# A convolution and two dense layers on one core: two accumulator readings awaited apart, and both layers' PSUM banks used in turn in the tail

## What is computed

```python
# attention-like part: a causal convolution of 7 taps, softmax weights per head (8 heads of 24 features)
x = attn(x, softmax(weight))                  # (2, 4096, 192) -> 8192 rows of 192
# layer 1
h = x @ w_in1                                 # 192 -> 2048
g = h * sigmoid(1.702 * h)
x = g @ w_out1                                # 2048 -> 192
# layer 2
h = x @ w_in2
P = a0 + a1*h + a2*h^2 + a3*h^3
Q = 1 + |b0|*|h| + |b1|*h^2
out = (P / (Q + 1e-6)) @ w_out2
```

## Time and profile before

| | |
|---|---|
| median of 3 runs | 1399.64 us (1399.02 to 1403.59) |
| the profiled execution's own time | 1398.76 us |
| its span in the trace | 1396.6 us, 2.2 us less than its time |
| PE busy | 1328.7 us, 95% of the span |
| DVE busy | 1107.6 us, 79% |
| ACT busy | 972.0 us, 70% |
| POOL busy | 326.5 us, 23% |

### The profile page before, as it was taken

How to read it: one execution, slowest core, us unless ns; L and a number is a source line. 1 busy time by engine, 2 the same in 40 slices (tenths; PEclk the granted TensorE clock), 3 DMA queues, 4 the chain that set the end, 5 groups by cost and what they waited for, 6 DMA issues and landing times. The chain is left out here.

```text
span 1396.6 us, 14941 instructions
## 1 busy us (share of the span) xinstructions
PE 1328.7 (95%) x4896; PEld 706.6 (51%) x4896; DVE 1107.6 (79%) x1205; ACT 972.0 (70%) x1113; POOL 326.5 (23%) x150
## 2 busy tenths in 40 slices
PE   2999999999999999999999999999999999999886
PEld 1455555554555555555554555555455555555332
DVE  5229788887888888888888888888888888877885
ACT  4337777677777777677777767777677777766774
POOL 4202222222222222222222222222222222222222
PEclk9999999999999999999999999999999999999998
DMA  8100000000000000000000000000000000000000
GB/s 209 36 12 0 12 1 23 1 23 1 12 11 0 23 0 20 3 11 11 0 23 0 12 10 3 20 0 23 0 12 12 0 12 1 12 0 12 0 12 11
DMA packets 32884, 20.37 MB, mean 15 GB/s; under 512 B 10322, under 2 KB 30802, under 8 KB 32850
## 3 DMA queue, kind: packets, MB, share of 16 engines
q1 hardware_dynamic: 32372, 19.93, 5.2%
q10 hardware_dynamic: 477, 0.01, 0.0%
HBM read 13.64 MB, written 6.29 MB: 14 GB/s over the span
## 5 line engine op out<-in xcount | busy, mean ns | idle before, releaser
L675 POOL TENSOR_TENSOR work<-work 128x1024 f32<-128x1024 f32 x128 | 303.7, 2373 | 1013.2 <-ACT work L432 1010.1
L271 PE MATMUL acc_a<-g,down 128*128 128x512 f32 x1024 | 477.4, 607 | 0.0
L271 PEld LDWEIGHTS acc_a<-g,down 128*128 128x128 f32 x1024 | 183.4, 190 | 292.5 <-issue 292.5
L570 DVE TENSOR_TENSOR work<-work,h 128x1024 f32<-128x1024 f32 x128 | 156.3, 1221 | 195.8 <-ACT work L432 195.7
L277 PE MATMUL acc_b<-g,down 128*64 128x512 f32 x1024 | 270.9, 606 | 30.0 <-DVE x_a_lo L588 16.0
L428 ACT ACTIVATE work<-h,par 128x1024 f32<-128x1024 f32 x128 | 142.6, 1114 | 195.8 <-PE h L265 195.8
L257 PE MATMUL h<-x_a_hi,up_a_hi 128*128 128x512 f32 x512 | 234.6, 458 | 25.4 <-DVE x_b L560 16.8
L456 ACT ACTIVATE work<-work 128x1024 f32<-128x1024 f32 x128 | 135.9, 1061 | 156.1 <-POOL work L675 154.1
L258 PE MATMUL h<-x_a_lo,up_a_hi 128*128 128x512 f32 x512 | 201.2, 393 | 0.0
L259 PE MATMUL h<-x_a_hi,up_a_lo 128*128 128x512 f32 x512 | 200.6, 392 | 0.0
L260 PE MATMUL h<-x_b,up_b_hi 128*128 128x512 f32 x512 | 200.4, 392 | 0.0
(11 more groups left out here) (74 smaller groups left out, 967.4 us busy)
## 6 DMA issues: line engine op xcount, KB each, us to landing
out<-y_out SPq DMA_DIRECT2D x16, 384.0 KB, 2.5
x_in_a<-in_x SPq DMA_DIRECT2D x16, 256.0 KB, 2.8
down<-in_moe_w_out SPq DMA_DIRECT2D x8, 384.0 KB, 6.3
x_in_b<-in_x SPq DMA_DIRECT2D x32, 64.0 KB, 2.6
work<-in_moe_w_in SPq DMA_DIRECT2D x8, 256.0 KB, 6.0
work<-in_moe_w_in SPq DMA_DIRECT2D x16, 128.0 KB, 6.3
wts<-in_weight ACTq DMA_DIRECT2D x2, 0.4 KB
wts<-in_weight SPq DMA_DIRECT2D x2, 1.3 KB
```

The source lines that it names most:

```text
L271: last = mm(l.acc_a[:], l.down[:, f, 0:P], l.g[:, slot, k, :], start=f == 0, stop=f == STEPS - 1)
L570: tt(tu, tu, h, ALU.mult).then_inc(t2_ready, 1)
L675: tt(m, sq[(s - LAG_RATIO) % 2], seed, ALU.mult).then_inc(m_ready, 1)
```

## The change

Two things are edited.

1. Once per tile, ahead of the down products, PE waits for one reading by ScalarE and one by VectorE only (counts 2i - 1, those of `acc_b`); the waits for both readings of `acc_a` (counts 2i) stand behind the products into `acc_b` and ahead of those into `acc_a`.
2. In the tail the hidden values of layer 2 go to `L1.h` in odd steps and to `L2.h` in even ones. From step 129 on PE's up product waits for `t3_ready` of one duo less. ScalarE's linear term L428 for the next duo is issued in step n instead of n + 1: behind step n's copies and ahead of L456. VectorE's L570 gets a wait for a new semaphore `t1_ready` in every step. GpSimd's product gets, in the tail, a wait for `z1_ready` (L594 of its own duo).

```diff
+        def alone(n):
+            return isinstance(n, int) and n >= TOTAL
+
+        def h2_banks(n):
+            return L1.h if alone(n) and n % 2 else L2.h
...
# TensorE, step n
                 if live(u):
...
-                    wait(pe, t3_ready, u)
-                    up(L2, d2, p2)
+                    if alone(n) and n > TOTAL:
+                        wait(pe, g1_ready, TOTAL)
+                        wait(pe, t3_ready, u - 1)
+                    else:
+                        wait(pe, t3_ready, u)
+                    up(L2, h2_banks(n), d2, p2)
...
                     if e1 == 0:
-                        wait(pe, x2_hi_done, 2 * i)
-                        wait(pe, x2_lo_done, 2 * i)
+                        wait(pe, x2_hi_done, 2 * i - 1)
+                        wait(pe, x2_lo_done, 2 * i - 1)
                     pe.wait_ge(g1_ready, v1 + 1)
                 if live(v2):
...
                     pe.wait_ge(g2_ready, v2 + 1)
                 for k in range(2):
                     if live(v2):
                         down_b(L2, e2, (s - LAG_DOWN2) % 2, k)
                     if live(v1):
                         down_b(L1, e1, (s - LAG_DOWN1) % 2, k)
                 if live(v1):
+                    if e1 == 0:
+                        wait(pe, x2_hi_done, 2 * i)
+                        wait(pe, x2_lo_done, 2 * i)
                     down_a(L1, e1, (s - LAG_DOWN1) % 2).then_inc(g1_used, 1)
...
# ScalarE, step n
+            def linear(n, k, slot):
+                act.wait_ge(h2_ready, k + 1)
+                wait(act, z1_ready, k - 1)
+                fn(t1[slot], h2_banks(n)[:], ACT.Identity, scale=scale_a3, bias=par[:, 2:3]).then_inc(t1_ready, 1)
...
                 if live(k):
...
-                    act.wait_ge(h2_ready, k + 1)
-                    wait(act, z1_ready, k - 1)
-                    fn(t1[(s - LAG_UP2) % 2], L2.h[:], ACT.Identity, scale=scale_a3, bias=par[:, 2:3])
+                    if not alone(n) or n == TOTAL:
+                        linear(n, k, (s - LAG_UP2) % 2)
                     wait(act, m_ready, k - 1)
-                    fn(sq[(s - LAG_UP2) % 2], L2.h[:], ACT.Square, scale=scale_root)
+                    fn(sq[(s - LAG_UP2) % 2], h2_banks(n)[:], ACT.Square, scale=scale_root)
                     wait(act, q_ready, k)
-                    fn(ab, L2.h[:], ACT.Abs, scale=scale_b0).then_inc(h2_read, 1)
+                    fn(ab, h2_banks(n)[:], ACT.Abs, scale=scale_b0).then_inc(h2_read, 1)
...
                 if s == S_X1 and tile_live(i + 1):
                     split_x1(i + 1, 1 - p)
+                if alone(n) and live(k + 1):
+                    linear(n + 1, k + 1, (s + 1 - LAG_UP2) % 2)
                 if live(v):
                     act.wait_ge(m_ready, v + 1)
                     wait(act, z2_ready, v)
                     fn(s1, m, ACT.Square, scale=root_c, bias=root_c * b1).then_inc(s1_ready, 1)
...
# VectorE, step n
                 if live(u):
+                    dve.wait_ge(t1_ready, u + 1)
                     dve.wait_ge(h2_read, u + 1)
                     tt(tu, tu, h, ALU.mult).then_inc(t2_ready, 1)
...
# GpSimd, step n
                     if live(v + 1):
                         pool.wait_ge(h2_read, v + 2)
+                    if alone(n):
+                        pool.wait_ge(z1_ready, v + 1)
                     wait(pool, s2_ready, v)
                     tt(m, sq[(s - LAG_RATIO) % 2], seed, ALU.mult).then_inc(m_ready, 1)
```

More of the change, by code:

```diff
@@ L159, in build_program @@
         x2_hi_done = sem("x2_hi_done"); x2_lo_done = sem("x2_lo_done")
-        h2_ready = sem("h2_ready"); h2_read = sem("h2_read")
+        h2_ready = sem("h2_ready"); h2_read = sem("h2_read"); t1_ready = sem("t1_ready")
         q_ready = sem("q_ready"); seed_ready = sem("seed_ready"); t2_ready = sem("t2_ready")
@@ L251, in _, with up @@
             mm = nc.tensor.matmul
-            def up(l, d, p):
+            def up(l, banks, d, p):
                 for k in range(2):
-                    h, cols = l.h[:, k, :], slice((2 * d + k) * P, (2 * d + k + 1) * P)
+                    h, cols = banks[:, k, :], slice((2 * d + k) * P, (2 * d + k + 1) * P)
                     mm(h, l.up_a_hi[:, cols], l.x_a_hi[:, p, :], start=True, stop=False)
@@ L260, in up, with up_rest @@
                     mm(h, l.up_b_hi[:, cols], l.x_b[:, p, :], start=False, stop=False)
-            def up_rest(l, d, p, k):
+            def up_rest(l, banks, d, p, k):
                 f, rows = 2 * d + k, slice(l.lo_row, l.lo_row + DB)
-                return mm(l.h[:, k, :], up_b_lo[rows, f * P:(f + 1) * P], l.x_b[rows, p, :], start=False, stop=True)
+                return mm(banks[:, k, :], up_b_lo[rows, f * P:(f + 1) * P], l.x_b[rows, p, :], start=False, stop=True)
             def down_a(l, d, slot):
@@ L324, in step @@
                     wait(pe, g1_ready, n)
-                    up(L1, s, p)
+                    up(L1, L1.h, s, p)
                 if live(u):
@@ L332, in step @@
                         pe.wait_ge(x2_lo_done, 2 * i)
-                    wait(pe, t3_ready, u)
-                    up(L2, d2, p2)
+                    if alone(n) and n > TOTAL:
[4 more added lines that the diff above has]
+                    up(L2, h2_banks(n), d2, p2)
                 for k in range(2):
                     if live(n):
-                        last1 = up_rest(L1, s, p, k)
+                        last1 = up_rest(L1, L1.h, s, p, k)
                     if live(u):
-                        last2 = up_rest(L2, d2, p2, k)
+                        last2 = up_rest(L2, h2_banks(n), d2, p2, k)
                 if live(n):
@@ L565, in step @@
                 u, v, t = n - LAG_UP2, n - LAG_RATIO, i - 1
-                h, tu, sk, zu = L2.h[:], t1[(s - LAG_UP2) % 2], sq[(s - LAG_UP2) % 2], z[(s - LAG_UP2) % 2]
+                h, tu, sk, zu = h2_banks(n)[:], t1[(s - LAG_UP2) % 2], sq[(s - LAG_UP2) % 2], z[(s - LAG_UP2) % 2]
                 zv, gv = z[(s - LAG_RATIO) % 2], L2.g[:, (s - LAG_RATIO) % 2, :, :]
                 if live(u):
+                    dve.wait_ge(t1_ready, u + 1)
                     dve.wait_ge(h2_read, u + 1)
```

## The result

The changed kernel takes 1437.8 us (median of 4 runs, 1436.4 to 1440.7) against 1400.3 us of the kernel before measured with it: a ratio of 1.027 (95% interval 1.0253 to 1.0287). It is slower, as forecast, and 12 us slower than forecast, near the upper end of the range. The profiled execution took 1440.65 us, span 1438.8 us.

A forecast was written before the change was run, and what follows sets the result against it. PE's queue bounds the steady part, a latency loop of PE, ACT and POOL the tail. 1398.76 - 10.5 (part 1) + 26.1 (loop) + 0 (end) + 10.4 (clock) = 1424.8, forecast as 1425.6 us; range 1411 to 1439.

The forecast's parts named there:

- The loop: Tail: L428 ahead of L456 closes a loop of 11.09 us per step against 8.36, +26.1 us in all.
- The step in which it starts: Tail, step 128: L456 waits behind the moved L428 and begins at 1303.19 instead of 1299.07.
- The clock: Tail, PE's stands of some 4.75 us: clock falls cost 2.61 us each, 8 times; half of 20.9 taken, +10.4 us.
- the second rival: Tail: the clock falls in every stand; 1436.1 us, up to 2.6 more if the last products are slow; chance 0.22.
- The end: Steps behind L456(136): last down products come 18.4 us after it, as before; 0 us.
- up to 2.6 more: Second rival's addition at the end: up to 2.6 us more if the last products are slow too.
- Part 1: Middle tiles: down products start after L585 instead of L588, 0.75 us per tile, 14 times, -10.5 us.
- The extra waits of DVE and POOL cost nothing: New waits for t1 and z1: t1 is written early, L594 ends about with L432; 0 us.

The follow-up runs named there:

- the clock held up: Changed kernel plus 15 added matmuls ahead of the down products of steps 129 to 132 and 135 to 137: 1421.1 us, ratio 1.015.
- part 1 alone: Kernel before with only the waits for the two accumulator readings split, nothing of the tail changed: 1389.5 us, ratio 0.991.

## Why the prediction was right, and where it was off

**The loop: right.** The step, that L428 stands ahead of L456 and blocks it, and that its `h` comes only behind down(n), which waits for the `g` of L456(n - 1), holds link by link: L439 waits for L273, L478 follows L439, PE waits 4.72 us for L608. Its length was 11.09 us by the rows of before and 11.08 us measured with the clock held up. Moving L428 alone (1395.0 us) and making `h` earlier alone (1387.0 us) each open it. The step in which it starts was +4.1 us, as laid out (4.6 against 0.5).

**The clock: the mis-sized term.** The sum took half of 20.9 us, "and I don't know that it comes in each". It came in each: eight steps took 108.0 us where the loop without it gives 8 x 11.09 + 1.4 = 90.1, so 17.9 us instead of 10.4. That is 1.9 to 2.4 us per fall and not 2.61: in the loop shown the clock came back 4.7 us after the down products had begun (the mean of 0.77 puts it at 1320.9), in the row of before 5.3 us (1384.5). The mechanism was that of the second rival. The Trainium skill ("TensorE: Matmul & The Clock Gate", section "HAM oscillation") had the clock fall ahead of every burst of its example; here it did in nine stands out of nine. The one row of before, one fall in one stand, had pointed the same way. That the second rival's 1436.1 us lies so near the measured time is in part luck: its clock term in the loop was 3.0 us too large, and 2.2 us of part 1 and 1.7 of the end make up for it. The range held because it had taken that rival in.

**The end: right in its place, off by the clock.** The last down products begin 1426.09 - 1407.63 = 18.46 us after L456(136), 18.4 forecast. From there to the end it is 12.7 us instead of 11.0, because the clock is low again (0.50 over 1428 to 1430); this was the "up to 2.6 more" of the second rival.

**Part 1: right in kind, 0.61 us instead of 0.75.** The step that failed is "The extra waits of DVE and POOL cost nothing". DVE's L593 starts 1.12 us after ACT's L452 starts, where L570 had started 1.06 us after L432 (727.64 - 726.52 against 726.98 - 725.92), and nothing hides that, since the tile's wait hangs on VectorE's chain. The rest is the release: PE goes 0.14 us after L608, and with part 1 alone, where nobody waits for t1, it also goes 0.14 us after `g`; I had taken 0.05 from the tail, up to 0.10 with the range of the start. In sum -8.3 us instead of -10.5. For POOL the sentence holds in the loop (108.06 us without its wait against 108.03) and not at the end, where leaving the wait out gave 3.2 us.

**What the forecast could not have:** the 4.7 us at the start of the profiled execution, which belong to no part of the change. Without them 1424.8 forecast stand against 1440.65 - 4.7 = 1435.9: of the 11.1 us missing, 7.5 are the clock in the loop, 1.7 the clock at the end and 2.2 part 1; the 0.3 too many are the difference between span and time, which is that much smaller after the change.

## What to carry to other kernels

Before moving an instruction up in an in-order queue, ask what its input waits for, and whether that waits for something now queued behind it: a prefetch whose operand comes one turn later in the other queue isn't a prefetch but a new link of the loop. Here the second pair of banks helped only once the producer's own queue was reordered with it (a step of 8.36 us became 13.3 with the consumer moved alone, 8.30 with neither moved and 7.46 with both). And where the list of waits gives a large sum, look at whether its end sets anything: 91.8 us of waiting on POOL had nothing to do with the loop's 108 us, though without it the end was 3.2 us shorter.

## What was not expected of the hardware

The clock fell in shorter stands than the 4.5 us of the row before. In the kernel with the linear term behind the seed it went from 1.00 to 0.50 within 1302 to 1303, in a stand of 1.84 us, 1.7 us after PE had stopped:

```profile
1301.00:1302.00 1.00, 0.19 (x1) 0.00 (x0) 0.91 (x2) 1.00 (x2) 0.00 (x0) 1.00 0.00 0
1302.00:1303.00 1.00, 0.00 (x0) 0.00 (x0) 1.00 (x2) 1.00 (x2) 0.00 (x0) 0.92 0.00 0
1303.00:1304.00 1.00, 0.97 (x2) 0.35 (x3) 1.00 (x1) 1.00 (x2) 0.00 (x0) 0.50 0.00 0
```

Two stands of 0.8 to 1.0 us per step had not done that in the kernel before, with the same work: its granted clock is 1.00 from 1300 to 1373. In this step the four products took 3.52 us instead of 1.93, and the step behind it 8.86 us instead of 8.30. The length of the stand alone doesn't tell: ahead of the down products of step 138 of the same execution PE stood 2.83 us, the granted clock read 1.00 throughout, and the four products took 1.93 us.

```profile
1372.00 1.93 PE L285 MATMUL acc_b<-g,down 128*64 128x512 f32 x4 [2.83 <-DVE g L608]
```

What decides between the two is not shown here. And PE had one of two starts for the same instructions: in two of 12 profiled executions its first products into `acc_b` took 3.67 us instead of 1.93, and the first mark came at 88.1 and 88.3 us instead of 83.0 to 83.8.
